# Attention in pairs of heads: one shared tile for two 64-query rests, four fills for q and k, the denominator's constant as a third sum

## What is computed

```python
# q, k, v: (2, 8, 1152, 64); 16 heads of 1152 rows
q_pool = q.reshape(B, H, S // 2, 2, D).mean(axis=3)          # 576 queries a head
scores = scale * np.matmul(q_pool, k.transpose(0, 1, 3, 2))  # 576 x 1152
scores = scores - np.max(scores, axis=-1, keepdims=True)
attn = np.exp(scores)
attn = attn / (np.sum(attn, axis=-1, keepdims=True) + 1e-09)
x = np.matmul(attn, v)
...
# then x goes through one gated feed-forward block (512 -> 1536 -> 512), and through
# eight experts (512 -> 1024 -> 512) weighed by a router with eight normalisations
```

## Time and profile before

| | us |
|---|---|
| median of 3 runs | 1288.01 (1287.23 to 1288.02) |
| the profiled execution | 1286.37, its span 1284.6 |
| PE busy | 1269.1 (99%) |
| DVE busy | 782.1 (61%) |
| ACT busy | 602.6 (47%) |
| POOL busy | 572.1 (45%) |

### The profile page before, as it was taken

The page is one execution under the profiler, slowest core; times in us unless marked ns, Lnnn a source line. Parts: engine busy times, 40 slices in busy tenths (PEclk is TensorE's granted clock), DMA queues, the critical chain, the costliest instruction groups (busy, mean ns, idle before and its releaser), DMA issues.

```text
span 1284.6 us, 20368 instructions
## 1 busy us (share of the span) xinstructions
PE 1269.1 (99%) x7788; PEld 1164.3 (91%) x7788; DVE 782.1 (61%) x1729; ACT 602.6 (47%) x1321; POOL 572.1 (45%) x355
## 2 busy tenths in 40 slices
PE   7999999999999999999999999999999999999999
PEld 6989999889999989989899999998999999999997
DVE  6999999993222314677566556556565475466443
ACT  6999998883333324444335234333233234234221
POOL 6377877770212247445235335335245246245211
PEclk9999999999999999999999999999999999999999
DMA  4334343202111043122123123122122122122112
GB/s 139 56 73 73 66 74 71 55 10 74 49 33 33 26 131 99 34 66 82 50 66 96 37 67 98 42 75 83 50 83 66 50 82 66 50 83 82 39 45 91
DMA packets 104091, 84.85 MB, mean 66 GB/s; under 512 B 14016, under 2 KB 80576, under 8 KB 104000
## 3 DMA queue, kind: packets, MB, share of 16 engines
q1 hardware_dynamic: 103712, 83.04, 24.0%
q10 hardware_dynamic: 288, 0.59, 0.2%
HBM read 79.15 MB, written 2.40 MB: 63 GB/s over the span
## 4 chain that ended last, share of the span: by engine, by line
PE 94%; DVE 4%; issue 0%; ACT 0%; DMA 0%; SPq 0%
PE bank L932 11%; PE bank L933 11%; PE bank L934 11%; PE bank L1086 10%; PE bank L1087 10%; PE bank L1088 10%; PE bank L775 6%; PE bank L794 6%; PE bank L909 4%; PE bank L911 4%; PE bank L910 4%; PE bank L803 3%; PE bank L804 3%; DVE part_min L1412 1%; PE bank L768 1%; DVE h_lo L1522 1%
## 5 line engine op out<-in xcount | busy, mean ns | idle before, releaser
L1531 DVE TENSOR_TENSOR c<-bank,c 128x256 f32<-128x256 f32 (+1 forms) x448 | 197.3, 456 | 282.7 <-PE bank L934 272.0
L714 POOL TENSOR_TENSOR w_lo<-w_raw,w_hi 128x1024 fp32r<-128x1024 f32 x64 | 153.9, 2405 | 300.4 <-ACT w_hi L1103 300.4
L1087 PE MATMUL bank<-w_lo,h_hi 128*128 128x512 f32 x576 | 225.0, 391 | 0.0
L1086 PE MATMUL bank<-w_hi,h_hi 128*128 128x512 f32 x576 | 225.0, 391 | 0.0
L1088 PE MATMUL bank<-w_hi,h_lo 128*128 128x512 f32 x576 | 224.3, 389 | 0.0
L1272 ACT ACTIVATE h_hi<-c 128x256 fp32r<-128x256 f32 (+1 forms) x256 | 112.7, 445 | 163.6 <-DVE c L1531 163.2
L1412 DVE TENSOR_REDUCE part_min<-bank 128x1 f32<-128x256 f32 (+2 forms) x240 | 122.1, 555 | 11.4 <-PE bank L804 8.4
L1088 PEld LDWEIGHTS bank<-w_hi,h_lo 128*128 128x128 f32 x576 | 108.2, 188 | 22.9
L1086 PEld LDWEIGHTS bank<-w_hi,h_hi 128*128 128x128 f32 x576 | 108.3, 188 | 20.7
L1087 PEld LDWEIGHTS bank<-w_lo,h_hi 128*128 128x128 f32 x576 | 108.3, 188 | 20.1
L1103 ACT ACTIVATE c<-bank 128x256 f32<-128x256 f32 (+1 forms) x64 | 26.2, 410 | 209.8 <-PE bank L934 209.8
(11 more groups left out here) (154 smaller groups left out, 3125.1 us busy)
## 6 DMA issues: line engine op xcount, KB each, us to landing
w_raw<-in_moe_w SPq DMA_DIRECT2D x64, 512.0 KB, 3.6
w_raw<-in_moe_w SPq DMA_DIRECT2D x64, 256.0 KB, 3.1
wo_raw<-in_moe_w_out SPq DMA_DIRECT2D x16, 384.0 KB, 3.4
v_raw<-in_v SPq DMA_DIRECT2D x16, 288.0 KB, 3.4
k_raw<-in_k SPq DMA_DIRECT2D x14, 288.0 KB, 8.5
q_raw<-in_q SPq DMA_DIRECT2D x15, 256.0 KB
gv_raw<-in_moe_w_gate SPq DMA_DIRECT2D x12, 256.0 KB, 2.9
gv_raw<-in_moe_w_val SPq DMA_DIRECT2D x12, 256.0 KB, 3.2
```

Of the source, the lines that this page charges most:

```text
L714: nc.gpsimd.tensor_tensor(w2_lo[:, u % 2], w2_raw[:], f32(w2_hi[:, u % 2]), ALU.subtract).then_inc(w2_split, 1)
L1086: nc.tensor.matmul(bank[:, 3 + i], hh, wh, start=first, stop=False)
L1087: nc.tensor.matmul(bank[:, 3 + i], hh, wl, start=False, stop=False)
L1531: nc.vector.tensor_tensor(dst[:, 0:w], bank[:, (u + b) % 3, 0:w], other[:, 0:w], ALU.add).then_inc(done, 1)
```

## The change

Two heads make a pair of nine tiles, i = 0 to 8, instead of ten. Tiles 0 to 3 are the even head's first 512 queries; tile 4 (`COMMON`) has the even head's last 64 queries in rows 0 to 63 and the odd head's first 64 in rows 64 to 127; tiles 5 to 8 are the odd head's other 512. In the shared tile both heads' matmuls run, each with zeros in the other's half, and sum in one bank. The zeros now come through `q_raw`, which has a sixth tile and halves zeroed once at the start. `pT_hi` and `pT_lo` become one tensor each, with both heads of a pair, and the copies of the shared tile write to both.

The 36 AV matmuls of the odd head before run in tiles 0 to 3, nine in each; those of the even head in tiles 4 to 8 (nine, nine, six, six, six). `AV_TILES` says how many tiles of the pair each half needs: 3 and 5 for the even head, 7 and 9 for the odd one. q and k come in four fills a head, of four, four, four and two transposes, in tiles 0 to 3 for the odd head and 5 to 8 for the next even one; the last has chunk 8 of k and tile 4 of q, and ACT copies it after both exponentials and `o_out`. `sums` gets a third column that holds EPS from the start, and `reciprocals` is left with two instructions. `k_first` is loaded through SP instead of ACT. POOL adds the query rows in one instruction over all five tiles. In the diff below, lines that only renumber waits are left out, and most removed lines too: they stand in the functions printed above.

```diff
 QT = 5
-QROWS = [128, 128, 128, 128, 64]
+PAIR = 9
+COMMON = 4
+FILLS = 4
...
-AV_UPTO = (9, 18, 24, 30, 36)
+AV_UPTO = (9, 18, 27, 36, 9, 18, 24, 30, 36)
...
-            pT_hi = pair("pT_hi", [PARTS, KCH, QLEN], F32R)
-            pT_lo = pair("pT_lo", [PARTS, KCH, QLEN], F32R)
+            pT_hi, pT_lo = allocate(s, [
+                ("pT_hi", [PARTS, 2, KCH, QLEN], F32R),
+                ("pT_lo", [PARTS, 2, KCH, QLEN], F32R)])
...
+                ("q_raw", [PARTS, QT + 1, 2 * DIM], F32),
...
-                ("sums", [PARTS, 2, QT, 2], F32),
+                ("sums", [PARTS, PAIR, 3], F32),
...
-        def pT_and_bank(dst, t, j):
-            r = QROWS[t]
+        def pT_and_bank(dst, i, j):
             c0, c1 = KEYS[j] // PARTS, KEYS[j + 1] // PARTS
-            return (dst[:, c0:c1, t * PARTS:t * PARTS + r],
-                    bank[:, 3 + j, 0:KEYS[j + 1] - KEYS[j]].rearrange("p (c n) -> p c n", c=c1 - c0)[:, :, 0:r])
+            src = bank[:, 3 + j, 0:KEYS[j + 1] - KEYS[j]]
+            if i == COMMON:
+                at = bass.AP(dst, c0 * QLEN + COMMON * PARTS,
+                             [[2 * KCH * QLEN, PARTS], [QLEN, c1 - c0], [KCH * QLEN - COMMON * PARTS, 2], [1, DIM]])
+                return at, src.rearrange("p (c a n) -> p c a n", c=c1 - c0, a=2)
+            a = i > COMMON
+            q0 = i * PARTS if not a else (i - COMMON - 1) * PARTS + DIM
+            return (dst[:, int(a), c0:c1, q0:q0 + PARTS], src.rearrange("p (c n) -> p c n", c=c1 - c0))
...
             def load_q(h):
-                to, done = (q_first, q_first_loaded) if h == 1 else (q_raw, q_loaded)
-                sp.dma_start(to[:, 0:4, :], q_dram[h][0:4 * PARTS].rearrange("(t p) n -> p t n", p=PARTS)).then_inc(done, 16)
-                sp.dma_start(to[0:QROWS[4], 4, :], q_dram[h][4 * PARTS:QLEN]).then_inc(done, 16)
+                a = h % 2
+                to, done = (q_first[:], q_first_loaded) if h == 1 else (q_tiles(a), q_loaded)
+                rest, rows, row0 = (0, slice(DIM, PARTS), 0) if a else (QT - 1, slice(0, DIM), 4 * PARTS)
+                sp.dma_start(to[:, a:a + 4], q_dram[h][DIM * a:DIM * a + 4 * PARTS].rearrange("(t p) n -> p t n", p=PARTS)
+                             ).then_inc(done, 16)
+                sp.dma_start(to[rows, rest], q_dram[h][row0:row0 + DIM]).then_inc(done, 16)
...
+            sp.dma_start(k_first[:], k_dram[1]).then_inc(k_first_loaded, 16)
             load_v(0)
...
-            def fill_kq(h, a, t, b):
...
+                if f == 0:
+                    pe.wait_ge(q_summed[h > 0], max(h, 1))
+                if f == 1:
+                    pe.wait_ge(k_split_done[h > 0], max(h, 1))
+                parts = ([(q_sum[a], i) for i in range(4)], [(k_split[a], i) for i in range(4)],
+                         [(k_split[a], i) for i in range(4, 8)], [(k_split[a], 8), (q_sum[a], 4)])[f]
+                for n, (src, i) in enumerate(parts):
+                    mm = nc.tensor.transpose(dst[:, n * PARTS:(n + 1) * PARTS],
+                                             f32(src[:, i]).rearrange("p a d -> p (a d)"), ident[:])
                 mm.then_inc(kq_filled, 1)
...
+            AV_TILES = ((3, 5), (7, 9))
...
+                        pe.wait_ge(v_split, h + 1)
+                    pe.wait_ge(p_lo_done, 3 * (PAIR * (h // 2) + AV_TILES[a][u]))
+                    if h == NHEAD - 1 and u == 1:
+                        pe.wait_ge(o_copied, 2 * h)
+                    elif (h >= 1 or u == 1) and h < NHEAD - 1:
+                        pe.wait_ge(o_copied, 2 * h + u)
+                src = (pT_lo if lo else pT_hi)
+                mm = nc.tensor.matmul(bank[:, o_bank(h, u), 0:QHALF], v_st[a][:, c], src[:, a, c, u * QHALF:(u + 1) * QHALF],
...
+            def score(i, j):
+                heads = (0, 1) if i == COMMON else (int(i > COMMON),)
+                for a in heads:
+                    t = i - COMMON * a
+                    qs = slice(t * PARTS, (t + 1) * PARTS)
+                    ks = k_st[a][:, KEYS[j]:KEYS[j + 1]]
+                    nc.tensor.matmul(scores(j), q_hi[a][:, qs], ks, start=(a == heads[0]), stop=False)
+                    mm = nc.tensor.matmul(scores(j), q_lo[a][:, qs], ks, start=False, stop=(a == heads[-1]))
+                mm.then_inc(s_ready, 1)
...
+            def next_kq(h, f):
+                if h < NHEAD:
+                    if f == 0:
+                        pe.wait_ge(kq_copied, FILLS * h)
...
+            def tile(g, pair, i):
+                h = 2 * pair + (i >= COMMON)
+                first, second = g == 0, g == 1
+                prev = (g + 1) % 2
+                if i in (0, COMMON):
+                    pe.wait_ge(q_lo_done, 2 * h + 1)
+                    pe.wait_ge(kq_copied, FILLS * h + 3)
+                if i in (COMMON, PAIR - 1):
+                    pe.wait_ge(q_lo_done, 2 * (2 * pair + i // (PAIR - 1)) + 2)
+                if not first:
+                    pe.wait_ge(exp_done, 2 * g - 1)
+                score(i, 0)
+                score(i, 1)
+                if i in (0, COMMON) and not first:
+                    pe.wait_ge(p_lo_done, 3 * g - 5)
+                    fill_p(prev, 0)
+                if not first:
+                    pe.wait_ge(exp_done, 2 * g)
+                if i in (0, COMMON):
+                    pe.wait_ge(kq_copied, FILLS * h + FILLS)
+                score(i, 2)
+                if i not in (0, COMMON):
+                    if not second:
+                        pe.wait_ge(p_lo_done, 3 * g - 5)
+                    fill_p(prev, 0)
+                if not first:
+                    if not second:
+                        pe.wait_ge(p_lo_done, 3 * g - 4)
+                    fill_p(prev, 1)
+                f = i if i < COMMON else i - COMMON - 1
+                if f in (0, 2, 3):
+                    next_kq(h + 1, f)
+                if h >= 1:
+                    for n in range(0 if i in (0, COMMON) else AV_UPTO[i - 1], AV_UPTO[i]):
+                        av(h - 1, n)
+                if not first:
+                    if not second:
+                        pe.wait_ge(p_lo_done, 3 * g - 3)
+                    fill_p(prev, 2)
+                if f == 1:
+                    next_kq(h + 1, f)
+            pe.wait_ge(const_done, 2)
 
 
...
+            def q_out(a, b, at, to):
+                return nc.scalar.activation(q_hi[a][:, to], bank[:, b, at], ACT.Copy, scale=-SCALE)
+            def kq_out(h, a, f, b):
+                act.wait_ge(kq_filled, FILLS * h + f + 1)
+                if f == 0:
+                    q_out(a, b, slice(0, 4 * PARTS), slice(0, 4 * PARTS)).then_inc(kq_copied, 1)
+                elif f < 3:
+                    copy(k_st[a][:, (f - 1) * 4 * PARTS:f * 4 * PARTS], bank[:, b]).then_inc(kq_copied, 1)
...
+                    copy(k_st[a][:, 8 * PARTS:SEQ], bank[:, b, 0:PARTS])
+                    q_out(a, b, slice(PARTS, 2 * PARTS), slice(4 * PARTS, QT * PARTS)).then_inc(kq_copied, 1)
...
+            def next_kq(h, f):
+                if h < NHEAD:
+                    kq_out(h, h % 2, f, 6)
+            def tile(g, pair, i):
+                h = 2 * pair + (i >= COMMON)
+                f = i if i < COMMON else i - COMMON - 1
+                act.wait_ge(nmax_done, g + 1)
+                for n, (k0, k1) in enumerate(EXP_KEYS):
+                    nc.scalar.activation(probs[g % 2][:, k0:k1],
+                                         columns[:, SCORES_AT[2 * n]:SCORES_AT[2 * n] + k1 - k0], ACT.Exp,
+                                         bias=nmax[:, i % QT:i % QT + 1], scale=-1.0,
+                                         accum_out=sums[:, i, n:n + 1]).then_inc(exp_done, 1)
+                if i in (1, 3, COMMON + 1, PAIR - 1) and h >= 1:
+                    o_out(h - 1, (h - 1) % 2, int(i in (3, PAIR - 1)))
+                if f in (0, 3):
+                    next_kq(h + 1, f)
+                if g >= 1:
+                    p_hi(g - 1, 2)
+                if f in (1, 2):
+                    next_kq(h + 1, f)
...
+            def q_lo_part(h, a, f, b):
+                dve.wait_ge(kq_copied, FILLS * h + f + 1)
+                cols = slice(0, 4 * PARTS) if f == 0 else slice(4 * PARTS, QT * PARTS)
+                src = bank[:, b] if f == 0 else bank[:, b, PARTS:2 * PARTS]
+                nc.vector.scalar_tensor_tensor(q_lo[a][:, cols], src, -SCALE, f32(q_hi[a][:, cols]),
                                                ALU.mult, ALU.subtract).then_inc(q_lo_done, 1)
...
             def reciprocals(h, a):
-                nc.vector.tensor_reduce(den[:, a], sums[:, a], AX.X, ALU.add).then_inc(den_step, 1)
-                dve.wait_ge(den_step, 2 * h + 1)
-                nc.vector.tensor_scalar(den[:, a], den[:, a], EPS, None, ALU.add).then_inc(den_step, 1)
-                dve.wait_ge(den_step, 2 * h + 2)
+                nc.vector.tensor_reduce(den[:, a], sums[:, COMMON * a:COMMON * a + QT], AX.X, ALU.add).then_inc(den_step, 1)
```

(36 more changed lines are left out.)

265 lines of the change are left out of this document (68 added, 197 removed).

## The result

The changed kernel takes 1293.19 us (median of five, 1292.81 to 1294.33) against 1288.01 us for the kernel before (1287.23 to 1288.42), a ratio of 1.0042 with a 95% interval of 1.0028 to 1.0057: 5 us slower. The forecast was 1301.0, 13 us slower. The sign held and the time lies in the range; the size was more than twice too large.

The account below looks back on a forecast made before the run. TensorE was busy 99%, with VectorE and ScalarE nearly level in attention, so instruction order decides. Seven pairs 13.2, first pair 0.3, last pair -0.9, start 0.2 make 12.8, say 13 us: 1301.0 from 1288.01, range 1290 to 1307.

Parts of the forecast that it names:

- the two AV waits: Even head's AV waits for `p_lo` two tiles back: 1.40 us in shared tile 4, 1.2 us in tile 6.
- tile 0: Pair's first tile: last fill, copied after both exponentials and `o_out`, delays the minima; 4.24 us, a wait of 0.57.
- tile 1: Pair's second tile: VectorE comes late, 0.76 us after scores began; k fill follows `q_lo`; 4.20 us, a wait of 0.6.
- the last pair: Last pair of heads: no fills in tiles 5 to 8, so 0.9 us less.
- start, with `k_first` on SP: Kernel start: `k_first` issued on SP's DMA queue ahead of `v` costs nothing to 0.6 us, taken as 0.2.
- first pair: First pair of heads: no AV before its fifth tile; 34.0 us against 33.7, 0.3 more.
- another tile's `p_lo`, and behind it the queue: Tiles 4 and 6: AV waits for `p_lo` issued after `nmax`; later matmuls, fills and scores wait behind; 1.40 and 1.2 us.
- The small addition: VectorE's 128x5 addition: 0.64 of its 0.81 us is a wait for GpSimd's shared ports that goes with the instruction.
- The shared tile's copies: Copies writing 64-column pieces into two heads' halves: between nothing and 0.3 us a copy, taken as nothing.
- The waits are covered: Rival: `p_lo` done before TensorE finishes its transposes, only work counts; 32.7 us a pair, 1273 us, 9%.
- Only the AV waits are real: Rival: slack absorbs ScalarE's late fill in i = 0 and 1; 35.3 us a pair, 1293.5 us, 13%.
- The rival of the costlier copies: Rival: 0.3 us for each of the shared tile's six copies and 0.5 more in i = 1; 1308 us, 6%.

Follow-up runs that it names:

- the same wait in the kernel before: Kernel before, with the first AV matmul of a head waiting for one tile more of `p_lo`: 1302.77 us, ratio 1.0116.
- the last arrangement of the AV matmuls: Changed kernel with odd head's AV matmuls over tiles 0 to 4, even head's over 5 to 8, last fill copied early: 1277.54 us, ratio 0.9923.

## Why the prediction was right and wrong

The mechanism was right for the two AV waits and for tile 0, and the size was wrong: 13 us forecast, 5.2 measured. The step that failed is tile 1, where the forecast had VectorE come out of tile 0 late, at 0.76 us, and the tile at 4.20; the runs showed no lateness at all, 0.52, and 3.88. That is 2 of the 7.8 us between 1301.0 and 1293.2. The small terms of the middle pairs make another 2, the last pair 1.5, the start and the first pair 0.6, and the profiled execution's distance to the median 1.6. That the time lies in the range is owed to the range's width, not to the sum.

In the trace the attention stage ended 6.7 us later than before (300.87 against 294.15), where the sum had 12.8; what follows took 990.53 and 990.45 us, untouched as forecast. The missing 6.1 us by part:

| | forecast | measured |
|---|---|---|
| start, with `k_first` on SP | +0.2 | -0.22 |
| first pair | +0.3 | +0.09 |
| six middle pairs | +11.3 | +7.33 |
| last pair and tail | +1.0 | -0.48 |

**The two AV waits: right.** 5.80 and 4.56 against 5.89 and 4.64, with 1.29 and 1.03 us idle. The step "another tile's `p_lo`, and behind it the queue" holds, and the same wait in the kernel before costs 15 us. Only the view that these waits are the price is too narrow: with its nine AV matmuls moved to a full tile, the first costs the same, in front of the fill. The hole is the shared tile's own, and AV matmuls that were ready would have filled it.

**Tile 0: right.** The fill is copied 1.16 us after the tile's start, as worked out, and the tile is 4.15 against 4.24.

**Tile 1: the step that failed, half of the middle pairs' miss.** I had VectorE come out of tile 0 at 0.76 us after the score's start, by adding up durations, and `nmax` at 2.31. The minima began at 0.52 (118.74) and `nmax` at 2.06 (120.28), the same as in a tile with no delay at all. In the kernel before VectorE did come late to this tile, with the addition in its queue (the score's start is 219.17):

```profile
220.13 1.48 DVE L1412 TENSOR_REDUCE part_min<-bank 128x1 f32<-128x256 f32 x3
```

That is 0.96 us after the start, and without the addition it was 0.52 there too. In after nothing of a lateness was left, and moving the fill forward didn't shorten the tile. From `nmax` on the forecast is right again: transposes 0.82 later, `q_lo` over 512 columns, then the k fill, 3.88. The durations were the error. I had 0.34 us for `q_lo`, and the minima started 0.21 after it; I had 1.94 from `nmax` to the next tile's minima, and it took 1.76 (116.98 to 118.74). With tile 1 starting 0.08 sooner that is 0.76 - 0.13 - 0.18 + 0.08 = 0.53. By the records an instruction of VectorE starts 0.06 to 0.09 us before the one ahead of it is through (118.28 with 0.52, then 118.74), unless it waits for a semaphore. The tile lost 0.32 us by this, 1.9 over six pairs. The other 2 us are small terms: 0.08 to 0.10 each in tiles 0, 4, 6 and 7 (tile 7 took 3.30 us, so its fourth k transpose was covered and not paid), and a pair before of 34.62, not 34.56.

**The last pair: a step that I hadn't taken.** I took the last pair of before for one like the others. It wasn't: its second tile took 4.05 us and its eighth 4.18, and up to its tenth tile it was 1.2 us longer than the pairs ahead of it. From the last tile's start to the end of the stage the changed kernel was 0.6 us shorter (10.82 against 11.45), where I had taken nothing. Against that its last pair took 0.4 more than forecast up to there, mostly in tile 6 (4.95). 1.2 + 0.6 - 0.4 are 1.4 of the 1.5 us.

**The start and the first pair.** `k_first` cost nothing on SP: the first score came 0.22 us earlier, not 0.2 later. The first pair took 33.84 us against 33.75 where I had 34.0 against 33.7; its first tile was over in 3.18.

**The profiled execution and the median.** 1.6 us of the distance between 1301.0 and 1293.2 is none of the kernel's doing: the profiled execution of before lies 1.6 us below its median, that of after at its own, and I had carried the gap over.

**The small addition: right.** *The Trainium skill, "SBUF — State Buffer", section "Who interferes with whom", has VectorE and GpSimd share a pair of ports under an exclusive lock that only some VectorE forms take. The traces agree:* a `TENSOR_SCALAR` on 128x5 ends with GpSimd's instruction (217.20 and 217.16), while the reciprocal behind it took its 0.19 us beside GpSimd's next instruction (217.22, and 217.12 with 1.43). The wait goes with the instruction, as forecast.

**The shared tile's copies: right at nothing.** The `p_lo` pair of instructions at 137.18, the second of which writes two heads' halves, lasts 1.01 us; two ordinary ones last 1.01 too (117.05).

**The rivals.** "The waits are covered" is what the last arrangement of the AV matmuls nearly reaches: 33.64 us a pair against the 32.7 that this rival had. "Only the AV waits are real", at 1293.5, names the measured time but not the cause: tile 0 kept its delay, 0.36 of which went when the fill was moved. The rival of the costlier copies was added up wrongly: six times 0.3 and 0.5 are 2.3 us a pair, not 0.9. Neither term came.

**What stays open.** In the kernels with the AV matmuls moved, and once each in the kernel before with the longer wait and without the addition, VectorE and ScalarE stood idle together for 0.4 to 2.1 us while TensorE's records ran on. Idle time of both says little by itself (after has 1.0 us behind each shared tile, up to the end of the transposes that both wait for); here what they wait for stands as finished. Every tile that this lengthened by 0.4 us or more was tile 3 or 8 of a pair or tile 3 of a head, in other pairs from one kernel to the next, and the times of one kernel scatter by up to 8 us. In the kernel before with only the addition changed:

```profile
38.58 0.71 PE L776 MATMUL bank<-ident,probs 128*128 128x128 f32 x5
...
41.26 0.49 ACT L1104 ACTIVATE pT_hi<-bank 128x384 fp32r<-128x384 f32 x1 [1.87 <-PE bank L776]
```

The transposes that ScalarE waits for are recorded as done at 39.29; the copy starts at 41.26. It looks like a signal of TensorE that arrives late. No run here tells where it was held up. The clock is not the cause: it was granted at 1.00 in every one of these tiles.

## What to carry over

In a loop in which three engines are level, ask of each wait what work stands behind it and whether other work is ready for the hole: moving nine AV matmuls away from their wait gained nothing where they came to stand in a full tile, and 1.4 us a pair (with the second wait) where they came to stand in tiles with idle time; putting ready ones into the hole gained 0.3 to 0.4 more. Take distances between starts, not durations, when a queue of eight short instructions is added up, and read the first and the last turn of a loop on their own, before too. Of a small instruction ask what runs beside it on the engine that it shares with: the same addition was worth 2.6 us in one order and 7 in another, 12.8 with the clock's falls. Read the granted clock of a stretch before two losses are taken for one kind.
